# Limiting the transfers in flight on the SP queue during the attention stage of an attention and mixture-of-experts kernel

## The chip, the cores and the metric

The kernel runs on 1 core of one Trainium2 chip. The metric is the device time of one execution in microseconds (us). Before the change three runs gave 517.41, 515.80 and 515.26 us; the median is 515.8 us.

## The reference, cut to what matters

Three layers follow one another: attention with a local window and block summaries, a mixture of 8 experts with one expert per token, and a dense layer with squared relu.

```python
# attention: B, H, S, D = 2, 8, 768, 64; block, window = 32, 16
k_sum = k.reshape(B, H, nb, block, D).max(axis=3)
v_sum = v.reshape(B, H, nb, block, D).mean(axis=3)
scores_l = scale * q @ k^T            # kept where |i - j| < window
scores_s = scale * q @ k_sum^T + log(block)
a = softmax(concat(scores_l, scores_s))
attn = a @ concat(v, v_sum)
# experts: 1536 tokens, 512 wide, 8 experts, 1024 hidden
e_idx = argmax(x @ w_gate + modality_bias[modality_id])
x = gate_w * (relu(x @ w1[e_idx]) @ w2[e_idx])
# dense: 512 -> 2048 -> 512
h = relu(x @ w_in);  out = (h * h) @ w_out
```

## The kernel before, in words

The program is written by hand, engine by engine, with semaphores between the engines. The attention stage takes about the first 75 us of the span. It works through NB = 12 blocks of 128 queries (6 for each of 2 batches). For block i, PE (TensorE) runs `scores(i)` (L1411, reads the query tile `q_in` and the key tile `k_in`), ACT the exponentials (L582), PE `turn(i)` (L1421, transposes of the probabilities) and `values(i)` (L1436, reads `v_in`), DVE `norm(i)` (L993, writes row block i of X). PE runs these software-pipelined: in turn i of its loop come `scores(i + 1)`, `x_turn(i - 3)` (L1445), `values(i - 2)`, `turn(i)`, and then the gate logits of an earlier block (L1451) at the head of the next `scores`. GpSimd (POOL) makes `k_in` from the batch's keys `kT` (L800) and from the block maxima `ksT` (L804), which DVE computes (`max_keys`, L936). DVE also sums the batch's values `vT` (`sum_values`, L962). Tile `vT` is the second half of X and is used for one batch after the other.

SP issues every load of the stage into one hardware queue, in an order written out by hand, and waits before a load only until its buffer is free. `q_in` has RING = 3 buffers, so the q of block i waits for `scores(i - 3)` (semaphore sc, L431). `v_in` has VRING = 4, so the v of block i waits for `values(i - 4)` (semaphore pv, L436). The second batch's vT waits until DVE has summed the first batch's (semaphore vtsum, L446). This text calls the loads by their block: q7 is the q of block 7, v4 the v of block 4. k10 to k13 are the four parts of the second batch's kT, and vTa and vTb are the two parts of its vT. A q is 256 KB, a v 390 KB, a part of kT 400 KB, a part of vT 768 KB. From q3 on the order is q3, v1, q4, k10, k11, k12, k13, q5, v2, v3, q6, vTa, vTb, v4, q7, v5, q8, two stores of zeros into the expert input (256 and 512 KB), v6, q9, a store of zeros, v7, q10, and so on. At the end of the stage SP also starts on the weights of the first expert (L458).

The rows of tokens that attention writes are scattered to DRAM by expert from GpSimd (L820) and the first expert tiles are read back (L842); the layers of the experts and the dense layer follow, on PE almost without a pause.

Of the kernel before, what the change touches and what calls it, by code (L numbers as in the profile page):

```python
# [21 lines left out]
NB = B * S // P  # L22
NBS = S // P
HALF = P // 2
PAIRS = H // 2
# [3 lines left out]
RING = 3  # L29
VRING = 4  # L30
# [5 lines left out]
N, DM, E, FE = B * S, H * D, 8, 1024  # L36
# [45 lines left out]
ZFIRST, ZSTEP = NBS - 1, 2  # L82
# [64 lines left out]
def build(nc, a):  # L147
# [170 lines left out]
    def wide(ap, axis, n):  # L318

        u = ap.unsqueeze(axis)  # L320
        shape = list(u.shape)
        shape[axis] = n
        return u.broadcast_to(shape)
# [14 lines left out]
    sem = {n: nc.alloc_semaphore("s_" + n) for n in names}  # L338
    s_q = [nc.alloc_semaphore(f"s_q{s}") for s in range(RING)]
    s_v = [nc.alloc_semaphore(f"s_v{s}") for s in range(VRING)]  # L340
    s_sum = [nc.alloc_semaphore(f"s_sum{s}") for s in range(RING)]
    s_kT = [[nc.alloc_semaphore(f"s_kT{b}{c}") for c in range(PAIRS)] for b in range(B)]
    s_vT = [[nc.alloc_semaphore(f"s_vT{b}{n}") for n in range(2)] for b in range(B)]
# [81 lines left out]
    with block:  # L425

        @block.sync
        def _(sp):
            def load_q(i):
                if i >= RING:  # L430
                    sp.wait_ge(sem["sc"], i - RING + 1)  # L431
                sp.dma_start(q_in[i % RING][:, :, :], a["q"][i]).then_inc(s_q[i % RING], 16)

            def load_v(i):
                if i >= VRING:
                    sp.wait_ge(sem["pv"], i - VRING + 1)  # L436
                sp.dma_start(v_in[i % VRING][NSUM:KEYS, :, :, :].rearrange("p a h d -> p (a h d)"), a["v"][i, :, 0:2 * H * (D + 1)]).then_inc(s_v[i % VRING], 16)

            def load_keys(b, c):
                sp.dma_start(kT[:, b, c, :], a["kT"][b, :, c, :]).then_inc(s_kT[b][c], 16)  # L440

            for c in range(PAIRS):
                load_keys(0, c)
            def load_values(b):
                if b:
                    sp.wait_ge(sem["vtsum"], PAIRS)  # L446
                for n in range(2):
                    pairs = slice(n * (PAIRS // 2), (n + 1) * (PAIRS // 2))
                    sp.dma_start(vT[:, pairs, :], a["vT"][b, :, pairs, :]).then_inc(s_vT[b][n], 16)
# [4 lines left out]
            def load_weights(e, part):  # L454
                for n in (part, part + 1):
                    w, k = (w1_v, KD // PARTS) if n < PARTS else (w2_v, KF // PARTS)
                    j = n % PARTS
                    sp.dma_start(raw[:, n * PW:(n + 1) * PW].rearrange("p (k f) -> p k f", k=k),  # L458
                                 w[bass.ds(e, 1), :, j * k:(j + 1) * k, :].rearrange("a p k f -> (a p) k f")
                                 ).then_inc(s_raw0[n], 16)  # L460
# [4 lines left out]
            load_values(0)  # L465
            load_v(0)
            load_q(3)
            load_v(1)
            load_q(4)
            for c in range(PAIRS):  # L470
                load_keys(1, c)
            load_q(5)
            load_v(2)
            load_v(3)
            load_q(6)
            load_values(1)
            for i in range(VRING, NB):
                load_v(i)
                if i + RING < NB:
                    load_q(i + RING)  # L480
                if i == ZFIRST:
                    sp.wait_ge(sem["zero"], 1)
                    sp.dma_start(xs_d[0:P, :], zero[:, :]).then_inc(sem["zfill"], 16)
                if ZFIRST <= i < ZFIRST + E // ZSTEP:
                    some = slice((i - ZFIRST) * ZSTEP, (i - ZFIRST + 1) * ZSTEP)
                    sp.dma_start(xs_d[P:, :].rearrange("(e r) d -> r e d", e=E)[0:P, some], wide(zero[:, :], 1, ZSTEP)
                                 ).then_inc(sem["zfill"], 16)
                if i == NB - RING:
                    sp.wait_ge(sem["e0"], 1)
                    e = sp.value_load(table[0:1, T_E0:T_E0 + 1], min_val=0, max_val=E - 1)  # L490
                    load_weights(e, 0)
# [1252 lines left out]
```

## Time and profile before

| | us |
|---|---|
| median of three runs | 515.8 |
| the three runs | 517.41, 515.80, 515.26 |
| the profiled execution, its own time | 518.67 |
| its span in the trace | 517.0 |
| PE busy in the span | 501.9 |
| DVE busy | 243.1 |
| ACT busy | 189.5 |
| POOL busy | 87.9 |

The profile is of one execution. Its own time, 518.67 us, is 1.7 us above its span and 2.9 us above the median of the three runs. Times in the trace are counted from the start of the span. A row of a timeline gives the start, the duration, the engine, the line and what was worked on, and in brackets how long the engine was idle before it and for what. "SPq" is SP's instruction queue: its rows are the issue of a transfer, not the transfer. A row "DMA to landing" gives the time from the start of the issue until the last of the 16 DMA engines has reported the transfer.

### The profile page before, as it was taken

To read this page: it belongs to the slowest core of one execution; us is meant where nothing else is said; L and a number is where in the kernel's file an instruction comes from. 1 tells how busy PE (TensorE), PEld (TensorE's weight loads), DVE (VectorE), ACT (ScalarE), POOL (GpSimd) and SP (SyncE) were. 2 spreads that over 40 slices of the span, in tenths; PEclk is the share of its full clock that TensorE was granted. 3 is DMA by queue.
4 is the path that set the end of the run, shared out by engine and by line. 5 is a ranking of instruction groups with operands and counts; after the bars stand their busy time and mean duration, and the time that the engine had idled before them with its cause. 6 is when DMAs were issued, how large, how long until landed. Compare 5 with 4: busy or idle time off the path is not lost.

```text
span 517.0 us, 9357 instructions
## 1 busy us (share of the span) xinstructions
PE 501.9 (97%) x3028; PEld 404.0 (78%) x3029; DVE 243.1 (47%) x449; ACT 189.5 (37%) x354; POOL 87.9 (17%) x110
## 2 busy tenths in 40 slices
PE   8899989999999999999999999999999999999995
PEld 4587878888788888787788888888888888888884
DVE  3787675978432657356542222732222273222221
ACT  1867665325522656334431221431221143122121
POOL 4534343117340040400000000020000011000002
PEclk9999989999999999999999999999999999999999
DMA  8999756275293449710400000140000001000002
GB/s 280 326 273 361 254 168 241 68 257 185 66 271 135 158 170 272 251 42 20 103 1 1 0 1 0 38 124 0 0 0 0 0 20 61 0 0 0 0 0 81
DMA packets 26926, 54.66 MB, mean 106 GB/s; under 512 B 2820, under 2 KB 13844, under 8 KB 26388
## 3 DMA queue, kind: packets, MB, share of 16 engines
q1 hardware_dynamic: 19108, 27.21, 18.1%
q0 software_dynamic: 5200, 23.62, 12.9%
q10 hardware_dynamic: 2592, 3.49, 1.9%
q8 instruction: 15, 0.25, 0.2%
q14 instruction: 11, 0.09, 0.1%
HBM read 42.24 MB, written 12.07 MB: 105 GB/s over the span
## 4 chain that ended last, share of the span: by engine, by line
PE 89%; DMA 5%; DVE 2%; issue 2%; ACT 1%; DVEq 0%; POOLq 0%; POOL 0%; ACTq 0%
PE psum L1692 8%; PE psum L1691 8%; PE psum L1693 8%; PE psum L1675 8%; PE psum L1677 8%; PE psum L1676 8%; PE psum L1577 5%; PE psum L1579 5%; PE psum L1578 5%; PE psum L1603 4%; PE psum L1601 4%; PE psum L1602 4%; DMA q_in<-in_q 3%; PE psum L1613 2%; PE psum L1496 2%
## 5 line engine op out<-in xcount | busy, mean ns | idle before, releaser
L1361 DVE TENSOR_TENSOR sq<-r_sb 128x512 f32<-128x512 f32 x48 | 33.2, 692 | 136.2 <-ACT r_sb L764 136.1
L764 ACT ACTIVATE r_sb<-psum 128x512 f32<-128x512 f32 x48 | 28.6, 597 | 144.9 <-PE psum L1677 144.9
L1675 PE MATMUL psum<-z_hi,W 128*128 128x512 f32 x192 | 75.9, 395 | 1.9 <-DVE W L1276 1.2
L1676 PE MATMUL psum<-z_lo,W 128*128 128x512 f32 x192 | 75.8, 395 | 0.0
L1677 PE MATMUL psum<-z_hi,W 128*128 128x512 f32 x192 | 75.8, 395 | 0.0
L1692 PE MATMUL psum<-W,s_hi 128*128 128x512 f32 x192 | 75.6, 394 | 0.0
L1691 PE MATMUL psum<-W,s_hi 128*128 128x512 f32 x192 | 75.6, 394 | 0.0
L1693 PE MATMUL psum<-W,s_lo 128*128 128x512 f32 x192 | 75.2, 392 | 0.0
L924 POOL DMA_INDIRECT out<-o_sb,sorted_m x12 | 11.6, 968 | 287.7 <-DVE o_sb L1381 285.2
L1363 DVE TENSOR_TENSOR s_lo<-sq,s_hi 128x512 fp32r<-128x512 f32 x48 | 33.3, 693 | 33.5 <-ACT s_hi L766 33.5
L1675 PEld LDWEIGHTS psum<-z_hi,W 128*128 128x128 f32 x192 | 36.0, 188 | 11.4 <-issue 1.6
L766 ACT ACTIVATE s_hi<-sq 128x512 fp32r<-128x512 f32 x48 | 30.3, 632 | 39.4 <-DVE sq L1361 39.4
L1577 PE MATMUL psum<-W,x_hi 128*128 (+1 forms) x104 | 42.3, 407 | 1.0 <-issue 1.0
L1677 PEld LDWEIGHTS psum<-z_hi,W 128*128 128x128 f32 x192 | 36.0, 187 | 8.7
L1691 PEld LDWEIGHTS psum<-W,s_hi 128*128 128x128 f32 x192 | 36.1, 188 | 8.5
L1676 PEld LDWEIGHTS psum<-z_lo,W 128*128 128x128 f32 x192 | 36.0, 187 | 8.5
L1693 PEld LDWEIGHTS psum<-W,s_lo 128*128 128x128 f32 x192 | 36.1, 188 | 8.2
L1692 PEld LDWEIGHTS psum<-W,s_hi 128*128 128x128 f32 x192 | 36.1, 188 | 8.1
L1601 PE MATMUL psum<-W,h_hi 128*128 (+1 forms) x104 | 42.1, 404 | 0.0
L1578 PE MATMUL psum<-W,x_hi 128*128 (+1 forms) x104 | 41.0, 395 | 0.0
L1579 PE MATMUL psum<-W,x_lo 128*128 (+1 forms) x104 | 41.0, 395 | 0.0
L1603 PE MATMUL psum<-W,h_lo 128*128 (+1 forms) x104 | 41.0, 394 | 0.0
(201 smaller groups left out, 736.4 us busy)
## 6 DMA issues: line engine op xcount, KB each, us to landing
raw<-in_w POOLq DMA_DIRECT2D x4, 2048.0 KB, 10.7
raw<-in_w_io POOLq DMA_DIRECT2D x4, 2048.0 KB, 8.5
v_in<-in_v SPq DMA_DIRECT2D x12, 390.0 KB, 12.9
raw<-in_w SPq DMA_DIRECT2D x8, 512.0 KB, 6.4
kT<-in_kT SPq DMA_DIRECT2D x8, 400.0 KB, 8.1
q_in<-in_q SPq DMA_DIRECT2D x12, 256.0 KB, 8.5
X<-in_vT SPq DMA_DIRECT2D x4, 768.0 KB, 12.3
ys_d<-y_sb ACTq DMA_DIRECT2D x12, 256.0 KB
```

The costliest lines, as they stand in the source:

```text
L1363: dve.tensor_tensor(s_lo[f % SBUFS][:, :], sq[:, :], s_hi[f % SBUFS][:, :].bitcast(F32), ALU.subtract).then_inc(sem["s_l"], 1)
L1577: pe.matmul(bank[h][:, :], x_hi[:, k, :], wh, start=(k == 0), stop=False)
L1578: pe.matmul(bank[h][:, :], x_hi[:, k, :], wl, start=False, stop=False)
L1579: ins = pe.matmul(bank[h][:, :], x_lo[:, k, :], wh, start=False, stop=(k == KD - 1))
L1601: pe.matmul(y, h_of(t)[1][:, k, :], wh, start=(k == 0), stop=False)
L1603: ins = pe.matmul(y, h_lo[:, k, :], wh, start=False, stop=(k == KF - 1))
L1675: pe.matmul(bank[f % 2][:, :], wh, z_hi[:, k, :], start=(k == 0), stop=False)
L1676: pe.matmul(bank[f % 2][:, :], wh, z_lo[:, k, :], start=False, stop=False)
L1677: ins = pe.matmul(bank[f % 2][:, :], wl, z_hi[:, k, :], start=False, stop=(k == KD - 1))
L1691: pe.matmul(bank[2 + j][:, :], s_hi[f % SBUFS][:, tok], wh, start=(f == 0), stop=False)
L1692: pe.matmul(bank[2 + j][:, :], s_hi[f % SBUFS][:, tok], wl, start=False, stop=False)
L1693: ins = pe.matmul(bank[2 + j][:, :], s_lo[f % SBUFS][:, tok], wh, start=False, stop=(f == KFF - 1))
```

## The change

SP gets more waits, and no instruction of any engine is moved. Two helpers, `q_landed` and `v_landed`, wait until the q or v of a block has landed. From v1 on, every load of the written order waits until a load a few places ahead of it has landed. Mostly this is the third ahead; v1, v4 and q7 wait for the second ahead (the first batch's second vT part, vTa and vTb), and v6 and the stores of zeros have waits that reach as far or further back. The waits for free buffers stay.

```diff
+            def q_landed(i):
+                sp.wait_ge(s_q[i % RING], (i // RING + 1) * 16)
+
+            def v_landed(i):
+                sp.wait_ge(s_v[i % VRING], (i // VRING + 1) * 16)
...
             load_q(3)
+            sp.wait_ge(s_vT[0][1], 16)
             load_v(1)
+            v_landed(0)
             load_q(4)
-            for c in range(PAIRS):
-                load_keys(1, c)
+            q_landed(3)
+            load_keys(1, 0)
+            v_landed(1)
+            load_keys(1, 1)
+            q_landed(4)
+            load_keys(1, 2)
+            sp.wait_ge(s_kT[1][0], 16)
+            load_keys(1, 3)
+            sp.wait_ge(s_kT[1][1], 16)
             load_q(5)
+            sp.wait_ge(s_kT[1][2], 16)
             load_v(2)
+            sp.wait_ge(s_kT[1][3], 16)
             load_v(3)
+            q_landed(5)
             load_q(6)
+            v_landed(2)
             load_values(1)
             for i in range(VRING, NB):
+                if i > VRING:
+                    q_landed(min(i + 1, NB - 1))
+                else:
+                    q_landed(6)
+                    sp.wait_ge(s_vT[1][0], 16)
                 load_v(i)
+                if i == VRING:
+                    sp.wait_ge(s_vT[1][1], 16)
+                else:
+                    v_landed(i - 1)
                 if i + RING < NB:
                     load_q(i + RING)
+                if ZFIRST < i < ZFIRST + E // ZSTEP:
+                    sp.wait_ge(sem["zfill"], (1 + i - ZFIRST) * 16)
```

The place that matters most below, on SP, from q6 to q8, before the change (X is vT here, the number behind q_in and v_in is the buffer's):

```order
L432 DMA q_in_62<-in_q 128x512 [waits s_sc]
L449 DMA X<-in_vT 128x1536 [waits s_vtsum]
L449 DMA X<-in_vT 128x1536
L437 DMA v_in_68<-in_v 96x1040 [waits s_pv]
L432 DMA q_in_63<-in_q 128x512 [waits s_sc]
L437 DMA v_in_69<-in_v 96x1040 [waits s_pv]
L432 DMA q_in_64<-in_q 128x512 [waits s_sc]
```

The same place with the change; the order is the same, and each load has a landing to wait for beside its buffer:

```order
L432 DMA q_in_62<-in_q 128x512 [waits s_sc,s_q2]
L455 DMA X<-in_vT 128x1536 [waits s_vtsum,s_v2]
L455 DMA X<-in_vT 128x1536
L437 DMA v_in_68<-in_v 96x1040 [waits s_pv,s_vT10,s_q0]
L432 DMA q_in_63<-in_q 128x512 [waits s_sc,s_vT11]
L437 DMA v_in_69<-in_v 96x1040 [waits s_pv,s_q0]
L432 DMA q_in_64<-in_q 128x512 [waits s_sc,s_v0]
```

The fifth row of both is q7: it now also waits for s_vT11, the landing of vTb.

## Rows read from the trace of the kernel before

**Rows 1.** The page: PE's share, and DMA's busy tenths in 40 slices.
```profile
PE 501.9 (97%) x3028; PEld 404.0 (78%) x3029; DVE 243.1 (47%) x449; ACT 189.5 (37%) x354; POOL 87.9 (17%) x110
...
DMA  8999756275293449710400000140000001000002
```

**Rows 2.** The chain of waits, 24 to 42 us: start, duration, what.
```profile
24.50 1.02 PE psum L1411 x32
...
25.55 15.24 DMA q_in<-in_q
...
40.92 1.05 PE psum L1411 x32
```

**Rows 3.** Timeline of SP's queue: v1, k10 to k13, q5, vTa/vTb, v4, q7.
```profile
12.09 0.43 SPq L437 DMA_DIRECT2D v_in<-in_v  x1
...
13.57 1.90 SPq L440 DMA_DIRECT2D kT<-in_kT  x4
16.68 0.33 SPq L432 DMA_DIRECT2D q_in<-in_q  x1
...
22.30 0.91 SPq L449 DMA_DIRECT2D X<-in_vT  x2
24.02 0.33 SPq L437 DMA_DIRECT2D v_in<-in_v  x1
25.55 0.33 SPq L432 DMA_DIRECT2D q_in<-in_q  x1
```

**Rows 4.** Landing of v1, issued at 12.1 us.
```profile
DMA to landing us min/median/max: 9.8/9.8/9.8
```

**Rows 5.** Landing of q5, issued at 16.7 us.
```profile
DMA to landing us min/median/max: 12.5/12.5/12.5
```

**Rows 6.** Landings of vTa and vTb, issued at 22.3 and 22.8 us.
```profile
DMA to landing us min/median/max: 13.1/14.7/16.2
```

**Rows 7.** Landing of v4, issued at 24.0 us.
```profile
DMA to landing us min/median/max: 16.0/16.0/16.0
```

**Rows 8.** Timeline of PE: values(1), scores(5), values(3), gate logits, scores(7).
```profile
26.00 1.15 PE L1436 MATMUL psum<-v_in,pT 120*64 120x65 f32 x32
...
29.34 1.39 PE L1411 MATMUL psum<-k_in,q_in 64*64 64x120 f32 x32
...
37.39 0.39 PE L1436 MATMUL psum<-v_in,pT 120*64 120x65 f32 x6 [0.24 <-issue]
...
39.17 1.06 PE L1451 MATMUL psum<-w_gate,xT 128*128 128x8 f32 x8 [0.37 <-ACT prob L582]
...
40.92 1.05 PE L1411 MATMUL psum<-k_in,q_in 64*64 64x120 f32 x32 [0.27 <-DMA q_in<-in_q]
```

**Rows 9.** Timeline of POOL: keys of the second batch's first block.
```profile
27.85 0.98 POOL L800 TENSOR_SCALAR k_in<-kT 128x384 f32<-128x384 f32 x2 [2.12 <-DMA kT<-in_kT]
33.06 0.35 POOL L804 TENSOR_SCALAR k_in<-ksT 128x192 f32<-128x192 f32 x1 [4.22 <-DVE ksT L936]
```

**Rows 10.** Timeline of DVE: maxima of k10 to k13, sums of vTa.
```profile
28.25 2.66 DVE L936 TENSOR_REDUCE ksT<-kT 128x24 f32<-128x768 f32 x3
...
32.03 0.95 DVE L936 TENSOR_REDUCE ksT<-kT 128x24 f32<-128x768 f32 x1
...
35.46 1.81 DVE L962 TENSOR_REDUCE vsT<-X 128x24 f32<-128x768 f32 x2 [1.45 <-DMA X<-in_vT]
```

**Rows 11.** Transfers of the page: KB each, us from issue to landing.
```profile
ys_d<-y_last SPq DMA_DIRECT2D x1, 256.0 KB, 2.1
```

**Rows 12.** Landing of the first part of kT, issued at 0.9 us.
```profile
DMA to landing us min/median/max: 4.4/4.4/4.4
```

**Rows 13.** Windows; the last three columns are PE clock, DMA share, GB/s.
```profile
21.00:26.00 5.00, 5.00 (x110) 3.86 (x102) 3.13 (x8) 3.25 (x11) 4.03 (x4) 1.00 1.05 376
26.00:31.00 5.00, 4.96 (x86) 4.20 (x86) 4.62 (x10) 3.59 (x11) 0.98 (x2) 1.00 1.04 250
...
39.00:44.00 5.00, 4.56 (x82) 3.73 (x83) 4.48 (x13) 3.50 (x12) 0.98 (x2) 1.00 1.04 380
```

## The prediction

> **What bounds the kernel now.** The page comes first: PE is busy 97% of the span, and the DMA engines are at nine tenths in a few of the first slices of 12.9 us, hardly later [rows 1]. The change touches SP alone, so it reaches the end only where PE waits for a load, or where a load holds up DVE or POOL and PE waits for those. The chain of waits shows the one such place. Scores of block 4 end at 25.52, q7 is issued at 25.55, takes 15.24 us to land at 40.79, and scores of block 7 start at 40.92 [rows 2]. That reads as if DMA bound these 15 us. The timeline of PE says otherwise: in that stretch PE stands only 0.24, 0.37 and 0.27 us, and once a group of score matmuls that takes 1.05 us elsewhere takes 1.39 [rows 8]. The stage is bound by PE's own work; q7 lands just as it is needed, 0.27 us late.
>
> Why does a 256 KB load take 15 us? Because SP issues far ahead. When q7 goes out at 25.55 [rows 3], q5, issued at 16.7, has not landed; it does at 16.7 + 12.5 = 29.2 [rows 5]. Eight loads are then in flight: q5, v2, v3, q6, vTa, vTb, v4, q7. They land in the order of issue: vTa at 22.3 + 13.1 = 35.4 and vTb at 22.8 + 16.2 = 39.0 [rows 6], v4 at 24.0 + 16.0 = 40.0 [rows 7], q7 at 40.8. So q7's 15 us are the time of the bytes ahead of it, and every load of this stretch is paced by bandwidth.
>
> **The change, part by part.** It adds waits to SP; no byte and no order changes. Waiting for the load three places ahead can't bring any load forward by itself, since what is ahead in the queue stays ahead. It can do harm where the queue runs dry before the next load is through its start-up.
>
> First, the steady run from v1 to vTb, with up to three loads in flight. From v1's landing at 12.1 + 9.8 = 21.9 [rows 4] to vTb's at 39.0 there are 11 landings in 17.1 us, so three take 4.7 us. A load issued when the third ahead has landed is in time if issue to landing takes no longer than this. The rows have two transfers of SP into an idle queue: 256 KB in 2.1 us (a store) [rows 11] and 400 KB in 4.4 us (the first load of all) [rows 12]. Both are below 4.7. I take 0 us for this part; its cover are the two loads in front. If the cover is short, as with the small q's, the upper end is 0.8 us for vTb, which is my estimate: about a third of the 2.3 us between the two rows, for one dry spot. The lower end is a gain, bounded below under the third rival.
>
> Second, what hangs on the single loads. v1 now waits for the first batch's vT, in flight since about 5 us, and moves from 12.09 [rows 3] to some 17 us. It lands at 21.9 before, and values(1) needs it at 26.00 [rows 8]: with 4.4 us it would be there. k10 waits for q3, and goes from 13.57 to about 20. DVE takes the maxima of k10 to k12 from 28.25 and of k13 at 32.03 [rows 10], long after the landings; POOL had its keys at 27.85, but then stood 4.22 us for DVE's maxima [rows 9], so a kT late by some 4 us is still hidden. q5 is not covered: it lands at 29.2 and scores(5) start at 29.34. vTa is not covered either: DVE stood 1.45 us for it at 35.46 [rows 10], and PE's idle 0.37 us at 39.17 follows from that. Both belong to the steady run, at 0 us.
>
> Third, q7, the one costed term. It may now be issued only when vTb has landed, at 39.0 instead of 25.55, and only v4 is in flight then (it waits for vTa, 35.4, which leaves it 4.6 us, so it still lands at 40.0). The lower bound is the idle queue's 2.1 us: 41.1, so +0.3 against 40.8. The upper bound of issue to landing is 4.4 us: 43.4, so +2.6. I take the 2.1 us and put v4's own 1.0 us (39.0 to 40.0) in front, because its data must pass first: 39.0 + 1.0 + 2.1 = 42.1, which is +1.3 us. 2.1 us and not 4.4, since q7 has the 2.1 us transfer's size and follows other loads, while the 4.4 us were taken by the first load of the program. PE waited for q7 before, so it passes on all of this.
>
> The Trainium skill has a price for this too, in DMA: Bandwidth & Descriptors, section Anatomy of one DMA: 2.0 us plus the bytes over 436 GB/s, fitted on GpSimd's path. By it 256 KB take 2.6 us; that estimate would put q7 at 41.6 and the kernel at 516.6. The same page, under Rules for kernel authors, tells one to issue early and wait late, which speaks against this change; the row of 15.24 us that cost PE 0.27 us agrees, and q7 issued at its last moment is what the rule warns of.
>
> Fourth, behind q7. v5 and q8 queue behind it on SP and come to land some 1 to 2 us after it, by 44. Scores(5) at 29.34 and scores(7) at 40.92 [rows 8] are two loop turns, 5.8 us each, so q8 is needed at about 46.7 and v5 later: hidden. The stores of zeros are only read by the scatter at the stage's end. From there on the loads are limited by free buffers, not by landings. The rest of the program moves with PE.
>
> Sum: 0 + 0 + 1.3 + 0 = **+1.3 us**. The profiled execution would go from 518.7 to 520.0; it is 2.9 us above the median of the runs, and I add the same 1.3 us to the median: 515.8 + 1.3 = **517.1 us**.
>
> **The rivals.** A measurement of this kernel can tell about 0.5%, or 2.6 us, from no change.
>
> *Nothing happens.* q7 lands near its lower bound and the steady run keeps up: +0.3 us or less, 515.8. For it speaks that every wait but q7's lies inside a queue that is some 10 us deep; against it, that PE has no slack at all for q7.
>
> *The queue runs dry, slower.* The place is q7 again, with the latency of the cold row: v4's 1.0 us and then 4.4 us give 44.4, +3.6 us, 519.4. The steady run may add to it, since q5 and vTa have no cover. It decides from q7 landing later than 43.4, which is 4.4 us after vTb: from there the change is slower by over 0.5%. For it speaks that the only load measured into an idle queue took 4.4 us; against it, that this load was the first of the program.
>
> *Fewer loads in flight move faster.* The engines moved 376 GB/s from 21 to 26 us, 250 from 26 to 31, 380 from 39 to 44, with a share of about 1 each time [rows 13]. Something slows them by a third for 5 us at a time. If it is that many loads are mixed on the 16 engines, a short queue ends it, all of the steady run lands earlier, and even a late issue of q7 is early enough. The gain is what PE stood: 0.34 (1.39 against 1.05) + 0.24 + 0.37 + 0.27 = 1.2 us [rows 8], 514.6. Against it: the fast window before 26 us has as deep a queue as the slow one. Over 0.5% it could only be if the slow stretches also cost PE, DVE and ACT time which the rows don't show as waits.
>
> **How the numbers follow.** Forecast, 517.1: 0.40. Nothing happens, 515.8: 0.20. Slower, 519.4: 0.25. Faster loads, 514.6: 0.15, of which 0.08 stay inside 0.5% and 0.07 go beyond, for that last reason. So faster 0.07; same 0.40 + 0.20 + 0.08 = 0.68; slower 0.25. The range takes in 514.6 and 519.4, each with the 0.6 us by which the lowest run lies below the median: 514.0 to 520.0. Outside are the larger gain and a steady run that falls behind as well, together under 2 in 10.
>
> **What would show it.** In the profile of the changed kernel SP's issue of q7 should stand just behind vTb's landing near 39 us, with q7 landing 2 to 4 us later instead of 15, and PE should stand 1 to 2 us before scores(7) for q_in where it stood 0.27. v1, k10 to k13 and q5 should land within 1 us of before. I would be wrong if PE stands for q5, if vTb lands over 1 us later (the run was not covered), or if vTb lands well before 39 and the windows at 26 to 31 and 34 to 39 us rise towards 380 GB/s: then the third rival holds.

## The result and the profile after

The changed kernel takes 522.8 us (median of five runs, 520.88 to 523.75) against 515.8 us (five runs, 515.26 to 517.89). The ratio is 1.0105 with a 95% interval of 1.0075 to 1.0134, so the change costs 3.9 to 6.9 us. The prediction was +1.3 us with a range up to 520.0 us. Its sign was right and its size wrong: the median rose by 7.0 us, and by the ratio it is 5.4 us.

The profiled execution has a span of 521.8 us against 517.0, +4.8 us. The page of the changed kernel, against [rows 1]:

```profile
PE 502.3 (96%) x3028; PEld 405.2 (78%) x3029; DVE 242.1 (46%) x449; ACT 189.7 (36%) x354; POOL 87.2 (17%) x110
...
PEclk9997998999999999999999999999999999999999
DMA  8888967266294249730400000050000001000002
```

The engines do the same work, and DMA is busy a little less in the first slices (8 for 9). Short windows show where. The last three columns are PE's clock, the share of the DMA engines that is busy (the mean of 16) and GB/s; first the changed kernel, then the kernel before:

```profile
17.00:19.00 2.00, 1.52 (x8) 0.78 (x8) 1.60 (x3) 1.75 (x6) 0.14 (x1) 1.00 0.41 87
32.00:34.00 2.00, 2.00 (x42) 1.93 (x43) 1.56 (x4) 1.85 (x7) 1.21 (x3) 1.00 0.71 171
39.00:42.00 3.00, 1.48 (x10) 1.01 (x10) 2.04 (x6) 2.82 (x10) 0.00 (x0) 0.98 0.28 82
```

```profile
17.00:19.00 2.00, 1.65 (x11) 1.11 (x12) 2.00 (x4) 1.75 (x6) 0.72 (x2) 1.00 1.03 260
32.00:34.00 2.00, 2.00 (x30) 1.93 (x27) 1.93 (x5) 2.00 (x9) 0.94 (x3) 1.00 1.06 382
39.00:42.00 3.00, 2.56 (x43) 1.97 (x44) 2.86 (x8) 2.10 (x7) 0.00 (x0) 1.00 1.06 391
```

The DMA engines now run short of work, most of all in these three stretches, where before they were busy throughout. The chain of waits of the changed kernel, from v2 to scores(8), start, duration and what:

```profile
26.88 4.95 DMA v_in<-in_v
...
31.85 0.35 SPq L455
...
32.24 8.84 DMA X<-in_vT
...
41.10 2.90 DMA q_in<-in_q
...
44.14 1.88 PE psum L1441 x32
46.02 1.04 PE psum L1475 x4
47.06 1.87 PE psum L1466 x32
```

Where the chain of before held one load, q7 [rows 2], it now goes through three in a row, each issued when the one in front of it in the chain has landed: v2, vTb, q7. vTb lands at 32.24 + 8.84 = 41.1 instead of 39.0, and q7 at 44.0 instead of 40.8. The timeline of PE shows what it paid, to be read beside [rows 8]:

```profile
31.88 1.15 PE L1466 MATMUL psum<-v_in,pT 120*64 120x65 f32 x32 [1.18 <-DMA v_in<-in_v]
...
39.89 1.06 PE L1481 MATMUL psum<-w_gate,xT 128*128 128x8 f32 x8 [0.95 <-ACT prob L612]
...
44.14 1.88 PE L1441 MATMUL psum<-k_in,q_in 64*64 64x120 f32 x32 [2.77 <-DMA q_in<-in_q]
45.95 1.11 PE L1475 MATMUL psum<-ident,X 128*128 128x128 f32 x4
46.99 1.94 PE L1466 MATMUL psum<-v_in,pT 120*64 120x65 f32 x32
...
51.68 1.05 PE L1441 MATMUL psum<-k_in,q_in 64*64 64x120 f32 x32
```

Two things are to be seen. PE stands (waits idle) for v2, for the exponentials (which wait on DVE, and DVE on vTa), and for q7. And behind the last stand the same matmuls take nearly twice as long: scores 1.88 us for 1.05, values 1.94 for 1.15. The windows give the reason:

```profile
40.00:45.00 5.00, 2.23 (x28) 1.79 (x31) 2.81 (x8) 1.82 (x6) 0.00 (x0) 0.69 0.52 176
45.00:50.00 5.00, 5.00 (x69) 4.25 (x62) 2.25 (x6) 2.90 (x10) 0.98 (x2) 0.63 1.04 361
50.00:55.00 5.00, 5.00 (x94) 4.18 (x92) 2.04 (x9) 2.73 (x9) 3.84 (x5) 1.00 1.02 311
```

PE's clock falls to its lower level, 1.2 of 2.4 GHz, at 41.9 us, when PE has stood for 0.5 us, and is back at 48.7 us. From 39 to 44 us it was 1.00 before [rows 13]. The Trainium skill tells of such a case in its page TensorE: Matmul & The Clock Gate, section "HAM oscillation — how this bites in real kernels": in a kernel in which each piece of compute was shorter than the DMA wait behind it, PE went back to half clock in the wait, and the next piece started cold. This trace agrees: between the stands of 0.95 and 2.77 us PE works 1.5 us (39.89 to 41.37), and scores(7) then take 1.88 us for 1.05.

This closes the account of the profiled execution to scores(8), which start at 51.68 against 46.39 before, +5.3 us:

| piece | us |
|---|---|
| vTb lands at 41.1 for 39.0 | +2.1 |
| q7 lands 2.9 us behind vTb for 1.8 | +1.1 |
| scores(7) to scores(8): 7.54 us for 5.47, half clock | +2.1 |

About 0.5 us of it comes back by the end, since the span grew by 4.8 us: the read of the first expert tile, on the path of both kernels, took 5.12 us in the chain after and 6.43 us before. How the loss divides among the pieces differs from run to run: in two later profiles with all the same waits (and idle matmuls on PE, below) vTb landed at 38.8 and 39.5 us and q7 at 43.7 and 42.6, but PE stood 1.86 and 2.12 us for the exponentials.

### The profile page after: what moved, and what is told of

Read it like the earlier page. It is cut to its first block, busy times and chain, and to the rows that moved or that the text cites. A ratio compares the mean times of both kernels' runs of the same rounds, so it can differ in the third digit from the quotient of the medians.

```text
span 521.8 us, 9376 instructions
## 1 busy us (share of the span) xinstructions
PE 502.3 (96%) x3028; PEld 405.2 (78%) x3029; DVE 242.1 (46%) x449; ACT 189.7 (36%) x354; POOL 87.2 (17%) x110
## 4 chain that ended last, share of the span: by engine, by line
PE 85%; DMA 9%; issue 2%; DVE 1%; SPq 1%; DVEq 0%; ACT 0%; POOLq 0%; POOL 0%; ACTq 0%
PE psum L1722 8%; PE psum L1721 8%; PE psum L1723 8%; PE psum L1705 8%; PE psum L1706 8%; PE psum L1707 8%; PE psum L1607 5%; PE psum L1608 5%; PE psum L1609 5%; PE psum L1631 4%; PE psum L1633 4%; PE psum L1632 4%; DMA v_in<-in_v 3%; PE psum L1643 2%; DMA X<-in_vT 2%
## 5 line engine op out<-in xcount | busy, mean ns | idle before, releaser
L1631 PE MATMUL psum<-W,h_hi 128*128 (+1 forms) x104 | 42.1, 405 | 0.0
L1608 PE MATMUL psum<-W,x_hi 128*128 (+1 forms) x104 | 41.1, 395 | 0.0
L1609 PE MATMUL psum<-W,x_lo 128*128 (+1 forms) x104 | 41.1, 395 | 0.0
```

What stands on the lines that cost most here:

```text
L1608: pe.matmul(bank[h][:, :], x_hi[:, k, :], wl, start=False, stop=False)
L1609: ins = pe.matmul(bank[h][:, :], x_lo[:, k, :], wh, start=False, stop=(k == KD - 1))
L1631: pe.matmul(y, h_of(t)[1][:, k, :], wh, start=(k == 0), stop=False)
```

## The experiments

All edits are to SP's order in the attention stage or to PE's idle matmuls. Kernels that ran together share one chip and its runs of the kernel before; ratios are against those. The median of the kernel before was 516.7, 521.5, 517.8 and 517.0 us in the four rounds, and much of the difference arises behind the attention stage (one profile has scores(8) where the changed kernel has them and a span 6.5 us longer), so the profiles are compared in the attention stage.

### Only the waits in front, only the waits behind

The first kernel keeps the waits from v1 to vTa and drops those in the loop from v4 on; the second does the reverse. The edit of the first:

```diff
             for i in range(VRING, NB):
-                if i > VRING:
-                    q_landed(min(i + 1, NB - 1))
-                else:
-                    q_landed(6)
-                    sp.wait_ge(s_vT[1][0], 16)
                 load_v(i)
...
```

> Only the added waits ahead of vTa and earlier (from v1 to vTa); from v4 on SP waits for free buffers alone. Theory A (the loss is v2 late by 1 us, then q7 issued only after vTb, then PE at half clock behind that stand): v2 still lands at about 31.8 us and PE stands 1.2 us for it; v4 and q7 sit in the queue behind vTb, so q7 lands about 1.5 us behind vTb (41), PE stands at most 2 us for it and the clock stays at 1.00: +1 to +2 us against the kernel before. Theory B (the queue runs dry everywhere and each wait costs its share): about half of the 5.4 us, +2.7, with later landings all through the stage.

> Only the added waits from v4 on; ahead of it SP waits for free buffers alone. Theory A: vTb lands at 39.0 as before, q7 is issued then and lands 2.9 us later at 42: PE stands about 1.5 us. If the clock stays at 1.00, +1.3 us; if it falls to 0.50 behind the stand as in the changed kernel, +3.4 us. Theory B: +2.7 us, in part from loads behind q8.

Measured: 1.0062 (1.0029 to 1.0094) with the front waits, 1.0056 (1.0021 to 1.0090) with the back ones. PE with the front waits alone:

```profile
41.92 1.88 PE L1470 MATMUL psum<-w_gate,xT 128*128 128x8 f32 x8 [3.52 <-ACT prob L601]
...
45.68 1.88 PE L1430 MATMUL psum<-k_in,q_in 64*64 64x120 f32 x32 [1.07 <-DMA q_in<-in_q]
```

vTa lands at 38.2 and vTb at 41.7 here, later than in the changed kernel, though v4, q7 and all behind wait for buffers alone. PE stands 3.52 us for the exponentials, which wait for DVE and vTa, and is at half clock already before q7. Theory A had named the front waits as worth 1 to 2 us and the clock as kept; both are wrong, +3.2 us by the ratio (1.5 to 4.9) and +4.5 us in the span. PE with the back waits alone:

```profile
42.91 1.57 PE L1428 MATMUL psum<-k_in,q_in 64*64 64x120 f32 x32 [1.42 <-DMA q_in<-in_q]
```

Here vTb landed at 38.3, q7 was issued then and landed 4.5 us later at 42.8, and the clock fell at 43.3 (scores(7) 1.57 us for 1.05). That is A's second case, +2.9 us by the ratio for its +3.4, though B's +2.7 fits as well. Each half costs about half of the whole.

### The one wait of the prediction's sum, alone and left out

```diff
 # the kernel before, with q7's wait alone
                 load_v(i)
+                if i == VRING:
+                    sp.wait_ge(s_vT[1][1], 16)
                 if i + RING < NB:
                     load_q(i + RING)
 # the changed kernel, without v4's and q7's waits
-                    sp.wait_ge(s_vT[1][0], 16)
                 load_v(i)
-                if i == VRING:
-                    sp.wait_ge(s_vT[1][1], 16)
-                else:
+                if i > VRING:
                     v_landed(i - 1)
```

> The kernel before with one wait more: q7 waits until vTb has landed. Theory A: the same as the kernel with all waits from v4 on, +1.3 us with the clock at 1.00 and +3.4 us with a fall to 0.50. Theory B: one wait of some forty costs next to nothing, 0 to +0.5 us.

> The changed kernel without two of its waits, that of v4 for vTa and that of q7 for vTb. Theory A: vTb lands at 41 as in the changed kernel, q7 2 us behind it at the latest instead of 3: PE stands 1 to 2 us for it instead of 2.8, the clock stays at 1.00, and the kernel is +1.5 to +2.5 us against before, so 3 us faster than the changed one. Theory B: as the changed kernel, +5 us.

The wait alone: 1.0021 (0.9988 to 1.0055), span 518.2 us, +1.2. Its timeline of PE, and q7's landing:

```profile
39.60 1.06 PE L1459 MATMUL psum<-w_gate,xT 128*128 128x8 f32 x8 [0.61 <-ACT prob L590]
...
41.88 1.05 PE L1419 MATMUL psum<-k_in,q_in 64*64 64x120 f32 x32 [0.80 <-DMA q_in<-in_q]
```

```profile
DMA to landing us min/median/max: 3.0/3.0/3.0
```

q7 goes out at 38.71 and lands 3.0 us later; PE stands 0.80 us and keeps its clock. The load takes what was predicted, nearly to the tenth; the time agrees but shows little, since the interval takes in 1. This kernel has no limit ahead of q7, and its DMA engines show what a wait for a landing meets:

```profile
36.00:39.00 3.00, 3.00 (x51) 2.41 (x44) 2.98 (x6) 1.16 (x4) 1.36 (x4) 1.00 0.14 42
```

vTb lands at 38.6 and v4 at 39.6, but from 36 to 39 us only 14% of the DMA engines' time is still busy. The 16 engines don't finish a load together, and it has landed when the last of them is through. With no wait the others can go on to the next loads meanwhile (the share stays at about 1 in the kernel before); with one they stand.

The opposite edit is a surprise: without v4's and q7's waits the changed kernel does not get faster, 1.0125 (1.0095 to 1.0155). SP issues q7 at 35.86, but vTb lands at 42.1, v4 at 43.4 and q7 at 45.6:

```profile
45.66 1.88 PE L1438 MATMUL psum<-k_in,q_in 64*64 64x120 f32 x32 [3.12 <-DMA q_in<-in_q]
```

So in the changed kernel taking q7's own wait away gives nothing back. With the run ahead of vTb late, q7 was late too, though it was issued 6 us before vTb's landing. Theory A falls. B's numbers, +2.7 us for each half and +5 here, came near; what takes its place is B with a reason, called C in the expectations below: with three in flight, a load's time from issue to landing is longer than the two ahead of it last.

### The depth of the queue

The front waits again, on the fifth load ahead and on the second instead of the third; nothing from v4 on. (In the changed kernel all the front waits, v1's too, are for the third load ahead: q3 and v0 stand between v1 and the vT part that it waits for.) For the fifth, against the kernel with the front waits:

```diff
-            sp.wait_ge(s_vT[0][1], 16)
+            q_landed(2)
             load_v(1)
-            v_landed(0)
+            sp.wait_ge(s_vT[0][0], 16)
             load_q(4)
-            q_landed(3)
+            sp.wait_ge(s_vT[0][1], 16)
             load_keys(1, 0)
...
-            v_landed(2)
+            sp.wait_ge(s_kT[1][3], 16)
             load_values(1)
```

> Waits from v1 to vTa as in the run that had only those, but each load waits for the fifth ahead instead of the third; from v4 on only free buffers. Theory C (with three in flight the issue to landing of each load is longer than the time the two in front last): with five in flight the four in front cover it, vTb lands at 38.5 to 39.5, v2 at 30.5, the clock stays at 1.00, and the time is that of the kernel before, within 0.3%. Rival D (any wait for a landing costs SP and the queue a fixed piece each): still +2 us or more, vTb after 40.

> The same with each load waiting for the second ahead. Theory C: two landings now take an issue to landing of about 4 us, 5 to 6 cycles for the 11 landings from v1 to vTb, so vTb lands at 44 to 46; PE stands for v2 and q5 too, and the time is +6 to +9 us. Rival D: no more than with three, +3 us.

The windows from 20 to 30 us, of the kernel before (no limit), with five, with three (the changed kernel) and with two in flight:

```profile
20.00:30.00 10.00, 10.00 (x190) 7.72 (x189) 7.64 (x18) 7.83 (x26) 5.01 (x6) 1.00 1.04 306
```

```profile
20.00:30.00 10.00, 9.78 (x190) 7.69 (x194) 7.61 (x17) 7.44 (x25) 5.01 (x6) 1.00 1.02 293
```

```profile
20.00:30.00 10.00, 10.00 (x196) 7.84 (x194) 7.82 (x18) 7.25 (x24) 5.01 (x6) 1.00 0.89 275
```

```profile
20.00:30.00 10.00, 9.12 (x163) 7.04 (x162) 7.67 (x17) 7.56 (x25) 4.04 (x4) 1.00 0.73 211
```

With five the DMA engines stay as busy as with no limit (1.02 and 1.04), with three they are busy 0.89 and with two 0.73 of the time. The other profiles agree: 1.04 or 1.05 in the five others without a limit in this stretch, 1.01 in the second with five, 0.81 to 0.86 in the four others with three. The stretch ends at 30 us because a longer one misleads. From 20 to 40 us the same four kernels move 302, 285, 261 and 213 GB/s, but the kernel with q7's wait alone moves 251, with no limit before 38.7 us and vTb on time: over 20 us the mean also counts loads and stores that are queued behind vTb.

vTb lands at 39.0, 38.1, 41.1 and 44.0, but by this single number the runs overlap: 37.6 to 39.0 in the four with the order of before and no front waits, 38.1 and 39.5 with five, 38.8 to 42.1 in the five with three. The packets of vTa and vTb in the traces tell it better. Nine tenths of them had started by 33.7 to 34.9 us in those four kernels, by 34.3 and 34.9 with five, by 36.7 to 38.7 in the five with three, and by 42.0 with two. With three in flight the bulk of the two loads was late in every profile, by some 2 to 5 us; the landing, that of the last engine, doesn't follow it closely. With two in flight PE stands 3.68 us for q5 already:

```profile
32.80 1.38 PE L1430 MATMUL psum<-k_in,q_in 64*64 64x120 f32 x32 [3.68 <-DMA q_in<-in_q]
```

That kernel measures 1.0115 (1.0060 to 1.0169), +6.0 us (3.1 to 8.8), at the lower end of C's +6 to +9; q5 issued at 29.3 lands in 3.3 us. Its ratio is of the three faster of only four runs (525.4 to 529.4 us), and its profile is of the slowest, 533.4 us. C's order of the depths holds, and D, a fixed price for each wait, does not: five and two have as many waits, and the kernel with five is not slower. The time of the kernel with five, 0.9966 (0.9936 to 0.9996), went against its profile, in which PE stands 1.34 us for q7 and runs at half clock behind it (scores(8) at 48.13). It was run again in the last experiment.

### The price of the clock

To see it by itself, PE ran idle matmuls where it stood for q7 in the changed kernel.

```diff
+                if i == NBS + 1:
+                    for _ in range(12):
+                        pe.matmul(s_bank(i, 0)[:, 0:PAIRS * KEYS], warm[:, 0:P], warm[:, 0:PAIRS * KEYS], start=True, stop=True)
                 mcol = CB["mask"][0] + kind * KEYS
```

> The changed kernel, and PE runs 12 idle matmuls of 128x480 bf16 (about 2.4 us, results overwritten) where it stands for q7. The loads are untouched. Theory C (the stand of PE costs twice: once as wait, once as half clock behind it): q7 lands as late as before (44), but scores(7), the x transposes and values behind it run at 1.05, 0.66 and 1.15 us instead of 1.88, 1.11 and 1.94, and the kernel comes to 2 us less than the changed one: about +3.3 us against the kernel before. Rival D (the clock is lost for another reason, such as the stand of 0.95 us before, or the matmuls delay q7's reader): same or slower than the changed kernel, +5.4 us or more.

Measured: 1.0145 (1.0078 to 1.0212), from only four runs (524.5 to 530.9 us). PE's timeline, and two windows:

```profile
40.72 1.06 PE L1484 MATMUL psum<-w_gate,xT 128*128 128x8 f32 x8 [1.86 <-ACT prob L612]
41.64 3.83 PE L1432 MATMUL psum<-warm 128*128 128x480 bf16 x12
...
46.20 1.05 PE L1444 MATMUL psum<-k_in,q_in 64*64 64x120 f32 x32
```

```profile
41.60:42.80 1.20, 1.20 (x8) 0.62 (x8) 1.20 (x3) 1.05 (x3) 0.00 (x0) 1.00 1.00 200
42.80:46.20 3.40, 3.40 (x10) 1.06 (x8) 0.75 (x5) 0.00 (x0) 0.00 (x0) 0.50 0.95 347
```

The experiment failed as a price. PE had stood 1.86 us just before. The 12 matmuls began at full clock; it fell 1.2 us into them, at 42.8, though PE was busy. They took 3.83 us instead of 2.4 (an estimate: 12 times 480 columns at 2.4 GHz), and PE came to scores(7) 2.5 us after q7's landing at 43.7. The real matmuls behind ran at full speed, but scores(8) started at 51.67, as without. What the clock gave back, the filling took. A second kernel filled the stand before too:

```diff
+                if i == NBS + 1:
+                    pe.wait_ge(sem["xtc"], NBS - 3)
+                    for _ in range(4):
+                        pe.matmul(bX[:, :], warm[:, 0:P], warm[:, :], start=True, stop=True)
                 if i >= 2:
```

> The changed kernel, and PE runs idle matmuls in both stands of block 7's turn: 4 of 128x512 where it stood 0.95 us for the exponentials, and 12 of 128x480 where it stood 2.77 us for q7. In the run with the 12 alone the clock had already fallen, and they took 3.8 us. Theory C (the half clock is the price of the two stands together, about 2 us): now the clock stays at 1.00, the 12 take 2.4 us, scores(7) start with q7's landing near 44 us and take 1.05 us, and scores(8) start near 49.7 us instead of 51.7. Rival D (the clock falls for another reason): the clock is again 0.5 from 42 on and scores(8) start near 51.7.

```profile
41.18 1.06 PE L1488 MATMUL psum<-w_gate,xT 128*128 128x8 f32 x8 [2.12 <-ACT prob L612]
42.10 4.28 PE L1436 MATMUL psum<-warm 128*128 128x480 bf16 x12
```

The four matmuls were too few: PE still stood 2.12 us, and the 12 took 4.28 us. The clock again fell at 42.8, 0.7 us into them. (The expectation says that it had fallen before the 12 matmuls; the windows show that it had not.) scores(8) came no sooner (52.18), and the kernel measured 1.0064 (1.0029 to 1.0099). Neither C nor D is decided by it: what the kernel would take with the same loads and the clock kept is not shown. The third try was at another place, the kernel before, where PE stands 1.62 us for the first expert tile at 73 us.

```diff
+                if isinstance(t, int) and t == 0:
+                    for _ in range(8):
+                        pe.matmul(x_bank(t)[:, :], warm[:, 0:P], warm[:, :], start=True, stop=True)
                 if isinstance(t, int) and t < 2:
                     pe.wait_ge(s_x0[t], 16)
```

> The kernel before, and PE runs 8 idle matmuls of 128x512 bf16 (about 1.7 us) where it stands 1.62 us for the first expert tile at 73 us. Theory C: the clock, 0.66 on average from 75 to 80 us before, stays at 1.00, the six first matmuls of the experts take 0.4 us and not 0.6, and the kernel is 1.5 us (0.3%) faster than before. Rival D: no change, or slower by what the idle matmuls overrun.

The first group of the experts in the kernel before, and the head of the second:

```profile
76.13 0.78 PE L1577 MATMUL psum<-W,x_hi 128*128 128x512 f32 x1
76.70 0.63 PE L1578 MATMUL psum<-W,x_hi 128*128 128x512 f32 x1
...
79.44 0.48 PE L1577 MATMUL psum<-W,x_hi 128*128 128x512 f32 x1
```

The same with the idle matmuls:

```profile
72.24 1.67 PE L1529 MATMUL psum<-warm 128*128 128x512 bf16 x7
...
75.84 0.47 PE L1580 MATMUL psum<-W,x_hi 128*128 128x512 f32 x1
...
78.11 0.48 PE L1580 MATMUL psum<-W,x_hi 128*128 128x512 f32 x1
```

Here the mechanism shows: with PE kept busy the first expert matmul takes 0.47 us for 0.78, and the second group starts 1.3 us sooner. The other traces bear it out. The clock fell behind this stand in the five profiles where PE stood 0.59 to 1.62 us, and in none of the six where it stood 0.36 us or less, nor in the three with the idle matmuls. The total did not follow: 1.0013 (0.9985 to 1.0040). By the last matmul of L1577 the lead was gone (229.3 us against 228.2, in profiles of different rounds); where it went was not tried.

### Looking for a version that beats both

Without any added wait, q6 and vTa were issued ahead of v3, and q7 ahead of v4; then the same with the 8 idle matmuls.

```diff
-            def load_values(b):
+            def load_values(b, parts=range(2)):
...
-                for n in range(2):
+                for n in parts:
...
             load_v(2)
-            load_v(3)
             load_q(6)
-            load_values(1)
+            load_values(1, (0,))
+            load_v(3)
+            load_values(1, (1,))
             for i in range(VRING, NB):
+                if i == VRING:
+                    load_q(i + RING)
                 load_v(i)
-                if i + RING < NB:
+                if VRING < i < NB - RING:
                     load_q(i + RING)
```

> The kernel before without any added wait, and SP's order changed at two places: q6 and vTa go ahead of v3, and q7 ahead of v4. Theory C (what counts is the place in the queue, not its depth): vTa lands about 0.6 us sooner (DVE's stand for it 0.8 instead of 1.45 us), q7 1 us sooner, PE's stands before scores(7) shrink from 0.9 us in sum to 0.3 or less, and the kernel is 0.5 us faster in its profile; in the median that can't be told from no change. Rival D (PE's stands there come from elsewhere): no change in the stands.

> The same order, and the 8 idle matmuls where PE stands for the first expert tile. Both gains together, 0.6 us and 1.3 us of clock: first expert matmuls of 0.4 us from the start, and 1.5 to 2 us (0.3 to 0.4%) faster than before. Rival D: within 0.2% of the kernel before.

Measured: 1.0006 (0.9970 to 1.0042) and 0.9993 (0.9963 to 1.0022). PE's stand before scores(7) in the first one:

```profile
36.33 1.03 PE L1439 MATMUL psum<-v_in,pT 120*64 120x65 f32 x26 [0.53 <-DMA v_in<-in_v]
38.08 0.39 PE L1439 MATMUL psum<-v_in,pT 120*64 120x65 f32 x6 [0.72 <-issue]
...
40.82 1.05 PE L1414 MATMUL psum<-k_in,q_in 64*64 64x120 f32 x32
```

vTa lands at 34.7 for 35.4 and the stand for the exponentials is gone. But v3, now behind vTa, lands at 36.3 and makes a stand of 0.53 us ahead of values(3), and one of 0.72 us within them (0.24 before) has no cause in the profile. q7 lands at 40.7, no sooner, and scores(7) start at 40.82 for 40.92. What the order gave one load it took from another. The span with both edits, 515.8 us, is the lowest of all profiles, but the ratio doesn't tell it from the kernel before.

> The waits for the fifth ahead from v1 to vTa, and the 8 idle matmuls where PE stands for the first expert tile. The run with the five alone measured 0.9966 of the kernel before, with 1 just outside its interval, while its profile had scores(8) 2 us later than a profile of the unchanged stage on the same chip. If five in flight is truly faster: 0.993 to 0.996 here, with the clock kept behind the stand. If that ratio was the spread of the measurement (theory C, which sees nothing to gain in a shorter queue): 0.999 to 1.003, and PE again stands over 1 us for q7 with the clock at 0.50 behind it.

This last kernel has the five in flight and the idle matmuls before the first expert tile (both edits as above). Measured: 0.9994 (0.9969 to 1.0018), and PE stood 0.81 and 0.48 us before scores(7), with half clock behind (values in 2.00 us for 1.15). Its vTb landed at 39.5. So the 0.9966 of the kernel with five was not met again, and no version here is shown to beat the kernel before.

## Why the prediction was wrong

**What bounds the kernel.** Right: PE's own work, with q7 landing just in time; and the place where the loss arises is the one named, scores(7). The count of eight loads in flight at 25.55 us leaves out k13, which landed at about 27.7; nothing hangs on it.

**First step, the steady run, 0 us: this failed.** It said that a load is in time if issue to landing takes less than three landings last, 4.7 us, and took 2.1 to 4.4 us for that from transfers into an idle queue. In the changed kernel the four parts of kT took 3.9 to 4.4 us, but v2 4.95 us, q6 5.1, v3 5.6 and vTb, of 768 KB, 8.8. From v1's landing at 21.2 to vTb's at 41.1 there are now 11 landings in 19.9 us for 17.1. The upper end given was +0.8 us for vTb; it was +2.1. Two loads in front were no cover: the DMA engines were busy 0.89 of the time from 20 to 30 us with three in flight, 1.02 with five and 1.04 with no limit. One reason is seen in the traces: the prediction treated the queue as one server, and a landing is that of the last of 16 engines, while the others stand if nothing more is issued (0.14 busy before vTb's landing in the kernel with q7's wait alone). How much is this and how much the start-up of each load was not separated. That q5 and vTa have no cover was seen, and v2 was the third: DVE waited for vTa 1.97 us instead of 1.45 [rows 10].

**Second step, the single loads.** Right for v1, k10 to k13 and q5: v1 landed at 21.2 and q5 at 28.8, both no later than before, and POOL waited for DVE as before [rows 9].

**Third step, q7, +1.3 us: right, with some luck.** 42.1 was worked out from vTb at 39.0, a load of 3.1 us; the kernel with this wait alone took 3.0 us, and its span was longer by 1.2 us. In the changed kernel it was 2.9 us. In three other kernels with the same wait it was 3.2, 4.5 and 4.8 us, so 3.1 is at the low end of what this load takes. The estimate of 2.6 us by the Trainium skill's page DMA: Bandwidth & Descriptors, section Anatomy of one DMA, whose fit is for GpSimd's path, was 0.3 to 0.4 us short of the two shortest.

**What the sum left out: the clock.** This failed too: no term stood for it, and nothing said why it should cost nothing. Scores(7) to scores(8) took 7.54 us for 5.47, +2.1 us, as much as vTb's delay; the score, transpose and value matmuls at half clock make up all of it (0.83 + 0.45 + 0.79). A row for it was in the trace: in the kernel before PE's first expert matmuls behind the stand at 73 us take 0.78 us and then 0.48. The upper end of the range lacked it too.

**Fourth step, behind q7.** Right: q8 landed at 46.0 and v5 at 45.4, in time.

**The rivals.** The second, that the queue runs dry, is what happened, in the steady run more than at q7. It had named the steady run only as an addition; the loads alone cost +3.2 us up to scores(7), near its +3.6, and the clock came on top. The third is refuted as a gain. Two of the windows that it named did rise, from 250 to 269 GB/s at 26 to 31 us and from 235 to 297 at 34 to 39, but 31 to 34 us fell from 379 to 189, and vTb landed later. That nothing happens is excluded by the interval.

## What to carry to other kernels

A queue that is full of loads looks like a long latency (15 us for 256 KB) and is none: as long as the bytes in front are needed sooner, its depth cost nothing here, while a limit of three loads, most of 256 to 400 KB, left the DMA engines idle for 11 to 19% of the time from 20 to 30 us; with five they stayed busy. A wait for a landing waits for the slowest of the 16 engines, so look at the DMA share just before a landing. A latency read off an idle queue is not the time that a load needs behind two others; read it where loads follow one another, or take the whole range. A mean rate over a stretch also counts loads that nobody waits for yet; compare when the loads that are needed get through. And a wait of PE is to be priced twice, once as the stand and once as the work behind it at half clock, if a row of the kernel shows the clock falling after a stand.

## What was not expected of the hardware

- The clock fell after stands that are hardly longer than others which it bore: 0.61 and 0.80 us before scores(7) left it at 1.00 (q7's wait alone), 0.81 and 0.48 us did not (five in flight, last run), nor did 0.41 and 1.34 us (five, first run). The lengths alone don't tell it. Nor does the clock always fall within a stand: it fell 0.4 to 0.8 us after PE was back at work in three kernels (the back waits, five in flight, last run), and 1.5 us after it at 75.0 us in the kernel before.
- Idle matmuls started behind a stand of 1.86 and of 2.12 us did not keep the clock. It fell 1.2 and 0.7 us into them, and they took 3.83 and 4.28 us for the estimated 2.4; so filling the second of two stands lengthened it.
- The 16 DMA engines can finish one load several us apart: nine tenths of the packets of vTa and vTb had started by 33.7 us in the kernel before, the last at 37.3, and vTb landed at 39.0.
- The rate of the loads swings between about 240 and 380 GB/s for some 5 us at a time in the kernel before [rows 13], at a DMA share of about 1 each time. What makes the swings stays open; the kernel with five in flight has them too (349 GB/s at 30 to 35 us, 205 at 35 to 39).
